# The low-order half of the attention scores as two 64-row matmuls in the two halves of the array

## The chip, the cores and the metric

The kernel runs on one core of a Trainium2 chip. The metric is the time of one execution on the device, in microseconds (us). A run of the kernel before is compared with runs of the changed kernel on the same chip; the profile is a trace of one execution. TensorE is called PE in the rows, its weight loads PEld, VectorE is DVE, ScalarE is ACT, GpSimd is POOL, and SP is the engine that issues most DMAs.

## The reference, cut to what matters

Three stages in a row: an attention with pooled queries, a mixture of eight experts with one expert for each token, and a gated feed-forward layer. The change touches the first alone.

```
B, H, S, D = 4, 8, 1152, 64
q_pool = q.reshape(B, H, S // 2, 2, D).mean(axis=3)        # 576 queries a head
scores = 1.0 / np.sqrt(D) * np.matmul(q_pool, k.transpose(0, 1, 3, 2))   # 576 x 1152
attn   = softmax(scores)                                   # over the 1152 keys
out    = np.matmul(attn, v)
```

## The kernel before

**Pairs and tiles.** The 32 heads are worked in 16 pairs. The 576 queries of each head are four tiles of 128 rows and a rest of 64; the two rests share a ninth tile. So a pair has nine score tiles: 0 to 3 of its first head, 4 to 7 of its second, and tile 8 (`TC`) with 64 rows of each. The 1152 keys are two halves of 512 columns (`h` 0 and 1) and a remainder of 128.

**Parts.** Each fp32 number is split into a high and a low part (fp32r), and a product is made from products of parts. For the scores, `kq_t` holds for each head 19 chunks of 128 columns: nine of keys, five of queries' high parts, five of queries' low parts. Its 128 partitions are two times 64: the keys' high parts lie in partitions 0 to 63 and their low parts in 64 to 127, and the query chunks stand in both halves alike. A score bank of 128 x 512 is then two matmuls over 128 rows in `scores` (L792): queries high by [keys high; keys low], then queries low by the same. Tile 8 has four a bank, two for each head. The remainder goes to bank R in the same way (`scores_rem`, L805). Three banks `S` hold the 18 halves of a pair in turn.

**Other work of a pair.** Transposes of the exponentials `probs` into three banks `T` (L694), from which ACT takes the high part `p_hi` (L514) and DVE the low part `p_lo` (L657); products of both with the values into bank O (L761, for tile 8 L770); groups of transposes of the next-but-one pair's keys and queries (`raw_k`, `q_sum`; also L694), whose parts ACT and DVE put into `kept_rows`; transposing matmuls of the result (L725). For each score half DVE takes a row maximum (L578), for each tile the negated maximum of all three parts (L591), then ACT takes the exponential with the row sum (L538).

**What sets the order.** All is written out by hand. `UNITS` is a list of 27 steps of a pair: b, a and c are transposes of `probs`, g the groups, x the results. `SCORES_AT`, `MAXIMA_AT` and `EXP_AT` say for each tile behind which step PE, DVE and ACT do its scores, maxima and exponentials. Every engine goes through the list in order. The products of a step come three steps behind its transposes. Before a half is written, PE waits until the exponential that read the same bank three halves earlier is done. SP's queue brings the parts from `kept_rows` to `kq_t` by `copy_parts` (L295, L297, L299: six DMAs a pair), then loads the keys, queries and values of the pair after next, then stores results.

The experts' gate logits, behind the attention, are the one place with small arrays: matmuls of 128 rows by 32 columns (L1353), and of 32 rows by 128 columns (L1363), between transposes (L1329).

Of the kernel before, what the change touches and what calls it, by code (L numbers as in the profile page):

```python
# [4 lines left out]
F32 = mybir.dt.float32  # L5
# [7 lines left out]
P = 128  # L13
# [48 lines left out]
def attention(nc, q, k, v, w_gate, w_out_gate, w1, x_dram, xs_dram, ys_dram, shared):  # L62
# [17 lines left out]
    B, H, SK, D = k.shape  # L80
# [4 lines left out]
    CH = SK // P  # L85
    QT = SQ // P
    REM = SQ - QT * P
    TILES = 2 * QT + 1
# [7 lines left out]
    HEAD = (CH + 2 * QC) * P  # L96
# [8 lines left out]
    SR = 3  # L105
# [4 lines left out]

    UNITS = [
# [3 lines left out]
    ]  # L115
    SCORES_AT = [(26, 26), (2, 2), (4, 5), (7, 8), (12, 13), (17, 17), (19, 20), (21, 22), (23, 24)]
    MAXIMA_AT = [(25, 25), (2, 2), (3, 4), (7, 8), (12, 13), (16, 16), (18, 19), (20, 21), (22, 23)]
    EXP_AT = [(0, 2, 2), (4, 4, 4), (7, 8, 8), (11, 11, 13), (16, 16, 17), (18, 19, 20), (21, 21, 21), (22, 23, 23), (25, 25, 25)]

    assert X_LOADS[X_EARLY - 1][1] * P <= (B - 1) * SQ and (B - 1) * HP <= LAST - 1  # L120
    assert w1.shape[2] == PIECE
# [51 lines left out]
    with ctx:  # L173
# [68 lines left out]
        KQ_DMAS, X_DMAS, COPIES = 6, 3, 3  # L242
        assert X_DMAS * PAIRS + 1 == X_STORES and x_out.shape[1] == TILES * D

        def sum_col(tile, part):
# [23 lines left out]
        with nc.Block() as block:  # L269

            @block.sync
            def _(sp):
# [18 lines left out]
                def copy_parts(par):  # L291

                    for h in range(2):
                        src, at = parts[h * D:h * D + D].bitcast(F32), h * HEAD
                        sp.dma_start(kq_t[par][0:D, at:at + HEAD].bitcast(F32), src[:, 0:LO_K]  # L295
                                     ).then_inc(kq_copied[h], 16)
                        sp.dma_start(kq_t[par][D:P, at:at + CH * P].bitcast(F32), src[:, LO_K:LO_K + CH * P]  # L297
                                     ).then_inc(kq_copied[h], 16)
                        sp.dma_start(kq_t[par][D:P, at + CH * P:at + HEAD].bitcast(F32), src[:, CH * P:LO_K]  # L299
                                     ).then_inc(kq_copied[h], 16)  # L300

                def store(p, kind):

# [387 lines left out]
            def _(pe):  # L691
# [82 lines left out]
                def operands(par, tile):  # L774

                    heads = (0, 1) if tile == TC else (tile // QT,)
                    at = CH + (QT if tile == TC else tile % QT)
                    return [(kq_t[par][:, h * HEAD + (at + part * QC) * P:h * HEAD + (at + part * QC + 1) * P], h)
                            for h in heads for part in range(2)]

                def scores(p, par, tile, h, opening=False):

                    if not (opening and 2 * tile + h < SR):

                        pe.wait_ge(exp_done, 2 * TILES * p + 2 * tile + h - SR + 1)
                    if tile in (0, QT) and h == 0:

                        pe.wait_ge(kq_copied[tile // QT], 16 * COPIES * (p + 1))
                    ops = operands(par, tile)
                    for n, (w, head) in enumerate(ops):  # L790
                        at = head * HEAD + h * 512
                        last = nc.tensor.matmul(S[(2 * tile + h) % SR][:, :], w, kq_t[par][:, at:at + 512],  # L792
                                                start=(n == 0), stop=(n == len(ops) - 1))
                    last.then_inc(s_ready, 1)

                def scores_rem(p, par, tile, opening=False):

# [11 lines left out]
                def body(p, par, kind):  # L809
                    j = 0  # L810
                    for n, step in enumerate(UNITS):
                        if step in steps(kind):
                            fill(p, par, kind, j, step)
                            done = lagged(kind, j)
                            if done is not None and is_prob(done):
                                products(p, par, kind, j - LAG, done)
                            j += 1
                        for tile in (*range(1, TILES), 0):
                            if kind == "tail" or (kind == "last" and tile == 0):
                                continue  # L820
                            of = (p, par) if tile else (p + 1, 1 - par)
                            opening = kind == "first" and tile > 0
                            if SCORES_AT[tile][0] == n:
                                scores(*of, tile, 0, opening)
                            if SCORES_AT[tile][1] == n:
                                scores(*of, tile, 1, opening)
# [10 lines left out]
                for g in range(GROUPS):  # L837
# [4 lines left out]
                scores(0, 0, 0, 0, True)  # L842
                scores(0, 0, 0, 1, True)
                scores_rem(0, 0, 0, True)
                over_pairs(pe, body)

# [997 lines left out]
```

## Time and profile before

| | us |
|---|---|
| three runs, lowest, median, highest | 1476.31, 1480.16, 1483.12 |
| the profiled execution | 1476.28 |
| its span, first to last instruction | 1474.5 |
| busy in the span: PE | 1377.8 |
| busy in the span: DVE | 873.2 |
| busy in the span: ACT | 638.4 |

The attention fills the first 600 us or so of the span. A matmul's duration in the rows is longer than the distance to the next, since matmuls are pipelined: how much time one takes on PE is read from start to start. The mean granted clock of TensorE was 0.981 of full speed, and 1.00 in the attention.

### The profile page before, as it was taken

To read this page: it belongs to the slowest core of one execution; us is meant where nothing else is said; L and a number is where in the kernel's file an instruction comes from. 1 tells how busy PE (TensorE), PEld (TensorE's weight loads), DVE (VectorE), ACT (ScalarE), POOL (GpSimd) and SP (SyncE) were. 2 spreads that over 40 slices of the span, in tenths; PEclk is the share of its full clock that TensorE was granted. 3 is DMA by queue.
4 is the path that set the end of the run, shared out by engine and by line. 5 is a ranking of instruction groups with operands and counts; after the bars stand their busy time and mean duration, and the time that the engine had idled before them with its cause. 6 is when DMAs were issued, how large, how long until landed. Compare 5 with 4: busy or idle time off the path is not lost. (4 is left out here: it accounts for less than half of the span.)

```text
span 1474.5 us, 24891 instructions
## 1 busy us (share of the span) xinstructions
PE 1377.8 (93%) x7733; PEld 1195.3 (81%) x7734; DVE 873.2 (59%) x1658; ACT 638.4 (43%) x1549; POOL 345.2 (23%) x241
## 2 busy tenths in 40 slices
PE   3999999999999999739978999998999999999998
PEld 2788888888888888537767787887999999999997
DVE  2899999999999998673443444445632323223232
ACT  2888888788888887532034102004411111111111
POOL 3122222222222220279179205022101010100000
PEclk9999999999999999969998999999999999999999
DMA  7566666666666764356256313114400000000000
GB/s 164 124 139 139 138 138 142 146 144 145 145 149 145 195 132 153 101 193 247 88 199 233 116 43 107 43 57 142 150 32 15 29 15 17 26 0 21 0 22 22
DMA packets 127931, 156.85 MB, mean 106 GB/s; under 512 B 47633, under 2 KB 86545, under 8 KB 125841
## 3 DMA queue, kind: packets, MB, share of 16 engines
q1 hardware_dynamic: 111968, 114.35, 30.8%
q10 hardware_dynamic: 12880, 31.99, 6.5%
q0 software_dynamic: 3040, 9.96, 2.0%
q8 instruction: 25, 0.41, 0.1%
q14 instruction: 18, 0.14, 0.0%
HBM read 87.33 MB, written 29.10 MB: 79 GB/s over the span
## 5 line engine op out<-in xcount | busy, mean ns | idle before, releaser
L514 ACT ACTIVATE p_hi<-ps_t 128x512 fp32r<-128x512 f32 (+1 forms) x336 | 194.3, 586 | 69.1 <-PE ps_t L694 64.7
L657 DVE TENSOR_TENSOR p_lo<-ps_t,p_hi 128x512 fp32r<-128x512 f32 (+1 forms) x336 | 216.9, 666 | 12.4 <-ACT p_hi L514 7.8
L578 DVE TENSOR_REDUCE maxima<-ps_s 128x1 f32<-128x512 f32 x288 | 193.7, 686 | 41.5 <-PE ps_s L792 37.7
L538 ACT ACTIVATE probs<-ps_s,neg_max 128x512 f32<-128x512 f32 x288 | 198.6, 690 | 44.1 <-DVE neg_max L591 43.9
L792 PE MATMUL ps_s<-kq_t 128*128 128x512 f32 x640 | 199.7, 414 | 13.6 <-DMA kq_t<-kept_rows 9.5
L694 PE MATMUL ps_t<-ident,probs 128*128 128x128 f32 x1296 | 198.5, 274 | 1.4 <-DVE kept_rows L569 0.8
L1026 POOL TENSOR_TENSOR w_parts<-raw_w,w_parts 128x1024 fp32r<-128x1024 f32 x64 | 150.9, 2396 | 184.5 <-ACT w_parts L1096 184.4
L694 PEld LDWEIGHTS ps_t<-ident,probs 128*128 128x128 f32 x1296 | 156.0, 140 | 46.3 <-DVE p_lo L657 9.6
L1642 ACT ACTIVATE silu<-ps_g 128x384 f32<-128x384 f32 x72 | 35.4, 491 | 314.6 <-PE ps_g L1748 314.6
L1695 DVE TENSOR_TENSOR silu<-ps_g,silu 128x384 f32<-128x384 f32 x72 | 40.1, 558 | 210.7 <-ACT silu L1642 210.7
L1096 ACT ACTIVATE w_parts<-raw_w 128x1024 fp32r<-128x1024 f32 x64 | 67.1, 1059 | 220.0 <-PE ps_h L1423 104.2
L761 PE MATMUL ps_o<-p_hi,v_hl 128*128 128x512 f32 x288 | 137.7, 478 | 8.4 <-DVE o_sb L598 5.2
L792 PEld LDWEIGHTS ps_s<-kq_t 128*128 128x128 f32 x640 | 114.7, 192 | 37.9 <-DMA kq_t<-kept_rows 9.9
L761 PE MATMUL ps_o<-p_lo,v_hl 128*128 128x512 f32 x288 | 113.6, 394 | 0.0
L1746 PE MATMUL ps_g<-mxt_hi,wg 128*128 128x384 f32 x288 | 97.5, 339 | 2.4 <-DVE mxt_lo L1670 2.4
L1748 PE MATMUL ps_g<-mxt_hi,wg 128*128 128x384 f32 x288 | 97.7, 339 | 0.0
L1747 PE MATMUL ps_g<-mxt_lo,wg 128*128 128x384 f32 x288 | 97.2, 338 | 0.0
L1421 PE MATMUL ps_h<-w_parts,xst_hi 128*128 x200 | 83.0, 415 | 14.6 <-POOL w_parts L1026 11.9
L1748 PE MATMUL ps_v<-mxt_hi,wv 128*128 128x384 f32 x288 | 96.4, 335 | 0.0
L1746 PE MATMUL ps_v<-mxt_hi,wv 128*128 128x384 f32 x288 | 96.4, 335 | 0.0
L1747 PE MATMUL ps_v<-mxt_lo,wv 128*128 128x384 f32 x288 | 96.4, 335 | 0.0
L1446 PE MATMUL ps_y<-w_parts,ht_hi 128*128 x200 | 81.7, 409 | 5.4 <-DVE ht_lo L1289 2.8
(190 smaller groups left out, 2786.5 us busy)
## 6 DMA issues: line engine op xcount, KB each, us to landing
raw_w<-in_moe_w ACTq DMA_DIRECT2D x61, 512.0 KB, 4.1
kq_t<-kept_rows SPq DMA_DIRECT2D x32, 608.0 KB, 6.2
kq_t<-kept_rows SPq DMA_DIRECT2D x32, 320.0 KB, 7.1
raw_k<-in_k SPq DMA_DIRECT2D x32, 288.0 KB, 5.7
raw_v<-in_v SPq DMA_DIRECT2D x16, 576.0 KB, 5.5
kq_t<-kept_rows SPq DMA_DIRECT2D x32, 288.0 KB, 6.5
raw_q<-in_q SPq DMA_DIRECT2D x32, 256.0 KB, 4.1
y_by_slot<-x_out SPq DMA_DIRECT2D x25, 256.0 KB, 2.0
```

The costliest lines, as they stand in the source:

```text
L514: nc.scalar.activation(p_hi[prob_ring(kind, m)][:, 0:w], T[ring(kind, j)][:, 0:w], ACT.Copy).then_inc(hi_ready, 1)
L538: nc.scalar.activation(probs[:, at:at + 512], S[(2 * tile + h) % SR][:, :], ACT.Exp, bias=neg_max[:, tile:tile + 1], accum_out=sums[par][: ...
L578: nc.vector.reduce_max(maxima[:, 3 * tile + h:3 * tile + h + 1], S[(2 * tile + h) % SR][:, :], AX).then_inc(max_done, 1)
L657: nc.vector.tensor_tensor(p_lo[n][:, 0:w], t[:, 0:w], p_hi[n][:, 0:w].bitcast(F32), ALU.subtract).then_inc(t_free, 1)
L694: last = nc.tensor.transpose(dst[:, n * P:(n + 1) * P], src, ident[:, :])
L761: last = nc.tensor.matmul(O[:, :], v_hl[v_par][:, c * P:(c + 1) * P], part[:, :], start=(i == 0 and n == 0), stop=(i == CH - 1 and n == 1))
L792: last = nc.tensor.matmul(S[(2 * tile + h) % SR][:, :], w, kq_t[par][:, at:at + 512], start=(n == 0), stop=(n == len(ops) - 1))
L1026: nc.gpsimd.tensor_tensor(w_part(n, parity, 1, at, PIECE), raw[j % RAW][:, :], w_part(n, parity, 0, at, PIECE).bitcast(F32), ALU.subtract) ...
L1421: nc.tensor.matmul(HB[h][:, :], xh, dyn(0, base, 0, at), start=(c == 0), stop=False)
L1746: nc.tensor.matmul(dst, wh, xh, start=(c == 0), stop=False)
L1747: nc.tensor.matmul(dst, wh, xl, start=False, stop=False)
L1748: last = nc.tensor.matmul(dst, wl, xh, start=False, stop=(c == DC - 1))
```

## The change

The second product (queries' low parts) needs the keys' high parts alone, 64 rows. `kq_t` is laid out anew: for keys 0 to 511 the high parts stay in partitions 0 to 63, for keys 512 to 1151 they lie in 64 to 127, and the low parts opposite. The second product of half 0 is then a matmul over rows 0 to 63 and that of half 1 over rows 64 to 127, into two different banks, issued one behind the other. Both halves of a tile are issued together, and PE's wait for a free bank stands before both. The copies become twelve DMAs a pair. `UNITS` and the three tables have new values. The product of the two low parts, which the kernel before also added, is left out in the 512-column halves.

```diff
     UNITS = [
         ("b", 0), ... ("b", 8),
-        ("g", 0), ("g", 1), ("c", 0), ("c", 1), ("c", 2), ("g", 2), ("a", 0), ("g", 3), ("a", 1),
-        ("a", 2), ("x", 0), ("a", 3), ("x", 1), ("a", 4), ("a", 5), ("a", 6), ("a", 7), ("a", 8),
+        ("g", 0), ("c", 0), ("c", 1), ("g", 1), ("g", 2), ("c", 2), ("g", 3), ("a", 0), ("a", 1),
+        ("a", 2), ("a", 3), ("x", 0), ("a", 4), ("x", 1), ("a", 5), ("a", 6), ("a", 7), ("a", 8),
     ]
-    SCORES_AT = [(26, 26), (2, 2), (4, 5), (7, 8), (12, 13), (17, 17), (19, 20), (21, 22), (23, 24)]
+    SCORES_AT = [26, 2, 5, 8, 12, 15, 17, 20, 23]
...
-                        sp.dma_start(kq_t[par][0:D, at:at + HEAD].bitcast(F32), src[:, 0:LO_K]
-                                     ).then_inc(kq_copied[h], 16)
-                        sp.dma_start(kq_t[par][D:P, at:at + CH * P].bitcast(F32), src[:, LO_K:LO_K + CH * P]
-                                     ).then_inc(kq_copied[h], 16)
-                        sp.dma_start(kq_t[par][D:P, at + CH * P:at + HEAD].bitcast(F32), src[:, CH * P:LO_K]
-                                     ).then_inc(kq_copied[h], 16)
+                        for rows, other, cols in ((slice(0, D), slice(D, P), slice(0, 512)),
+                                                  (slice(D, P), slice(0, D), slice(512, CH * P))):
+
+                            sp.dma_start(kq_t[par][rows, at + cols.start:at + cols.stop].bitcast(F32), src[:, cols]
+                                         ).then_inc(kq_copied[h], 16)
+                            sp.dma_start(kq_t[par][other, at + cols.start:at + cols.stop].bitcast(F32),
+                                         src[:, LO_K + cols.start:LO_K + cols.stop]).then_inc(kq_copied[h], 16)
+                        for rows in (slice(0, D), slice(D, P)):
+                            sp.dma_start(kq_t[par][rows, at + CH * P:at + HEAD].bitcast(F32), src[:, CH * P:LO_K]
+                                         ).then_inc(kq_copied[h], 16)
...
-                def scores(p, par, tile, h, opening=False):
+                def scores(p, par, tile, opening=False):
 
-                    if not (opening and 2 * tile + h < SR):
+                    if not (opening and 2 * tile + 1 < SR):
 
-                        pe.wait_ge(exp_done, 2 * TILES * p + 2 * tile + h - SR + 1)
+                        pe.wait_ge(exp_done, 2 * TILES * p + 2 * tile + 1 - SR + 1)
...
                     ops = operands(par, tile)
-                    for n, (w, head) in enumerate(ops):
-                        at = head * HEAD + h * 512
-                        last = nc.tensor.matmul(S[(2 * tile + h) % SR][:, :], w, kq_t[par][:, at:at + 512],
-                                                start=(n == 0), stop=(n == len(ops) - 1))
-                    last.then_inc(s_ready, 1)
+                    first, second = ops[:len(ops) // 2], ops[len(ops) // 2:]
+                    banks = [S[(2 * tile + h) % SR] for h in range(2)]
+                    for h in range(2):
+                        for n, (w, head) in enumerate(first):
+                            at = head * HEAD + h * 512
+                            nc.tensor.matmul(banks[h][:, :], w, kq_t[par][:, at:at + 512], start=(n == 0), stop=False)
+
+                    for n, (w, head) in enumerate(second):
+                        for h in range(2):
+                            rows, at = slice(h * D, h * D + D), head * HEAD + h * 512
+                            last = nc.tensor.matmul(banks[h][:, :], w[rows, :], kq_t[par][rows, at:at + 512],
+                                                    start=False, stop=(n == len(second) - 1))
+                            if n == len(second) - 1:
+                                last.then_inc(s_ready, 1)
```

In the rows of order, names carry their buffer number, and REGISTER_ALU, L715 and the like only work out the value of a wait. The first place is PE around score tile 3 of a pair in the loop. Before, the two banks are filled behind two different steps:

```order
L694 MATMUL ps_t0<-ident,probs 128x128 x4
L761 MATMUL ps_o<-p_hi6,v_hl0 128x512
L761 MATMUL ps_o<-p_lo6,v_hl0 128x512
L785 REGISTER_ALU
L792 MATMUL ps_s0<-kq_t1 128x512 x2
L706 REGISTER_ALU
L694 MATMUL ps_t1<-ident,probs 128x128 x4
L761 MATMUL ps_o<-p_hi0,v_hl0 128x512
L761 MATMUL ps_o<-p_lo0,v_hl0 128x512
L785 REGISTER_ALU
L792 MATMUL ps_s1<-kq_t1 128x512 x2
```

And with the change, behind one step (L799 is the first product over 128 rows, L804 the second over 64):

```order
L698 MATMUL ps_t1<-ident,probs 128x128 x4
L765 MATMUL ps_o<-p_hi0,v_hl0 128x512
L765 MATMUL ps_o<-p_lo0,v_hl0 128x512
L789 REGISTER_ALU
L799 MATMUL ps_s0<-kq_t1 128x512
L799 MATMUL ps_s1<-kq_t1 128x512
L804 MATMUL ps_s0<-kq_t1 128x512
L804 MATMUL ps_s1<-kq_t1 128x512
```

The four matmuls stay four; they stand together now, and the 64-row ones are enclosed by 128-row work on both sides. The second place is PE from score tile 5 to score tile 6. Before:

```order
L694 MATMUL ps_t1<-ident,probs 128x128 x4
L792 MATMUL ps_s1<-kq_t1 128x512 x2
L785 REGISTER_ALU
L792 MATMUL ps_s2<-kq_t1 128x512 x2
L706 REGISTER_ALU
L694 MATMUL ps_t2<-ident,probs 128x128 x4
L761 MATMUL ps_o<-p_hi0,v_hl1 128x512
L761 MATMUL ps_o<-p_lo0,v_hl1 128x512
L706 REGISTER_ALU
L725 MATMUL ps_t0<-stack2,o_sb 128x64 x4
L785 REGISTER_ALU
L792 MATMUL ps_s0<-kq_t1 128x512 x2
```

With the change, from the last matmul of tile 5 to the first of tile 6:

```order
L804 MATMUL ps_s2<-kq_t1 128x512
L710 REGISTER_ALU
L715 REGISTER_ALU
L698 MATMUL ps_t0<-ident,probs 128x128 x4
L710 REGISTER_ALU
L698 MATMUL ps_t1<-ident,probs 128x128 x4
L774 MATMUL ps_o<-v_hl0,p_hi6 128x256
L774 MATMUL ps_o<-v_hl0,p_lo6 128x256
...
L789 REGISTER_ALU
L799 MATMUL ps_s0<-kq_t1 128x512
```

Between the two tiles there are now two steps (the rows left out are two more pairs of L774), and tile 6 starts with a wait for tile 5's first exponential where before it was for tile 4's second. The third place is SP's queue in one pair, before:

```order
L295 DMA kq_t<-kept_rows 64x2432
L297 DMA kq_t<-kept_rows 64x1152
L299 DMA kq_t<-kept_rows 64x1280
L295 DMA kq_t<-kept_rows 64x2432
L297 DMA kq_t<-kept_rows 64x1152
L299 DMA kq_t<-kept_rows 64x1280
L275 ISA
L275 DMA raw_k<-in_k 128x9x64
```

And with the change:

```order
L298 DMA kq_t<-kept_rows 64x512
L300 DMA kq_t<-kept_rows 64x512
L298 DMA kq_t<-kept_rows 64x640
L300 DMA kq_t<-kept_rows 64x640
L303 DMA kq_t<-kept_rows 64x1280 x2
L298 DMA kq_t<-kept_rows 64x512
...
L303 DMA kq_t<-kept_rows 64x1280 x2
L275 ISA
L275 DMA raw_k<-in_k 128x9x64
```

The bytes are the same; the loads of keys and queries now stand behind twelve DMAs in place of six.

## Rows read from the trace of the kernel before

**Rows 1.** Busy time of each engine in a stretch of the attention
```profile
core 0: us, PE busy (x) PEld busy (x) DVE busy (x) ACT busy (x) POOL busy (x), PEclk, DMA share, GB/s
170.00:240.00 70.00, 69.22 (x447) 58.90 (x445) 64.75 (x134) 57.46 (x158) 13.86 (x12) 1.00 0.63 142
```

**Rows 2.** Timeline of PE, one step with score tile 3: start, us, operation
```profile
208.65 0.60 PE L694 MATMUL ps_t<-ident,probs 128*128 128x128 f32 x4
209.00 0.48 PE L761 MATMUL ps_o<-p_hi,v_hl 128*128 128x512 f32 x1
209.32 0.40 PE L761 MATMUL ps_o<-p_lo,v_hl 128*128 128x512 f32 x1
209.56 0.63 PE L792 MATMUL ps_s<-kq_t 128*128 128x512 f32 x2
210.02 0.60 PE L694 MATMUL ps_t<-ident,probs 128*128 128x128 f32 x4
```

**Rows 3.** Timeline of PE, the same place in two pairs that follow each other
```profile
204.44 0.50 PE L761 MATMUL ps_o<-p_hi,v_hl 128*128 128x512 f32 x1 [0.26 <-DVE o_sb L598]
...
239.92 0.50 PE L761 MATMUL ps_o<-p_hi,v_hl 128*128 128x512 f32 x1 [0.27 <-DVE o_sb L598]
```

**Rows 4.** Timeline of the weight loads, two that follow each other
```profile
208.98 0.19 PEld L761 LDWEIGHTS ps_o<-p_hi,v_hl 128*128 128x128 f32 x1
209.09 0.19 PEld L761 LDWEIGHTS ps_o<-p_lo,v_hl 128*128 128x128 f32 x1
```

**Rows 5.** Timelines of PE, weight loads and DVE, from 32-column to 32-row matmuls
```profile
632.92 0.28 PE L1353 MATMUL ps_h<-w_parts 128*32 128x256 f32 x1
...
633.13 0.18 PEld L1363 LDWEIGHTS ps_l<-stack,h_sb 32*128 32x128 f32 x1 [0.21 <-issue]
...
631.95 0.67 DVE L1168 COPY h_sb<-ps_h 32x512 f32<-32x512 f32 x1
```

**Rows 6.** Timeline of the weight loads, from 32-row matmuls back to full transposes
```profile
628.26 0.30 PEld L1363 LDWEIGHTS ps_l<-stack,h_sb 32*128 32x128 f32 x2
628.59 0.20 PEld L1329 LDWEIGHTS ps_tx<-ident,x_half 128*128 128x128 f32 x2
```

**Rows 7.** Timelines of PE and weight loads, from 32-column matmuls to full transposes
```profile
625.93 0.86 PE L1353 MATMUL ps_h<-w_parts 128*32 128x512 f32 x3
626.63 0.27 PE L1329 MATMUL ps_tx<-ident,x_half 128*128 128x128 f32 x1
...
626.39 0.38 PEld L1329 LDWEIGHTS ps_tx<-ident,x_half 128*128 128x128 f32 x2
```

**Rows 8.** Groups of DVE and ACT in the attention: busy us, mean ns of one
```profile
L578 DVE TENSOR_REDUCE maxima<-ps_s 128x1 f32<-128x512 f32 x288 | 193.7, 686 | 41.5 <-PE ps_s L792 37.7
L591 DVE TENSOR_REDUCE neg_max<-maxima 128x1 f32<-128x3 f32 x144 | 22.5, 156 | 5.0
L538 ACT ACTIVATE probs<-ps_s,neg_max 128x512 f32<-128x512 f32 x288 | 198.6, 690 | 44.1 <-DVE neg_max L591 43.9
```

**Rows 9.** Waits in the attention: engine, line, waited for, us in total, times, longest
```profile
PEld ps_s L792 <- ACT probs L538: 8.4, 8, 1.5
PE ps_s L792 <- ACT probs L538: 3.9, 5, 0.8
```

**Rows 10.** Timeline of PE in the opening of the first pair
```profile
28.89 2.24 PE L792 MATMUL ps_s<-kq_t 128*128 128x512 f32 x4 [0.82 <-ACT probs L538]
31.89 2.24 PE L792 MATMUL ps_s<-kq_t 128*128 128x512 f32 x4 [0.77 <-ACT probs L538]
```

**Rows 11.** Timelines of SP's queue, POOL and PE: copies, their use, the next loads' use
```profile
220.78 0.49 SPq L295 DMA_DIRECT2D kq_t<-kept_rows  x1
...
221.96 2.42 SPq L299 DMA_DIRECT2D kq_t<-kept_rows  x1
...
227.58 2.48 SPq L299 DMA_DIRECT2D kq_t<-kept_rows  x1
...
241.20 0.72 POOL L420 TENSOR_TENSOR q_sum<-raw_q 64x64 f32<-64x64 f32 x2
...
238.13 1.09 PE L792 MATMUL ps_s<-kq_t 128*128 128x512 f32 x4
...
246.88 0.60 PE L694 MATMUL ps_t<-ident,raw_k 128*128 128x128 f32 x4
```

More of the change, by code:

```diff
@@ L112, in attention @@
         ("b", 0), ("b", 1), ("b", 2), ("b", 3), ("b", 4), ("b", 5), ("b", 6), ("b", 7), ("b", 8),
[2 rows of a table removed]
-    ]
-    SCORES_AT = [(26, 26), (2, 2), (4, 5), (7, 8), (12, 13), (17, 17), (19, 20), (21, 22), (23, 24)]
-    MAXIMA_AT = [(25, 25), (2, 2), (3, 4), (7, 8), (12, 13), (16, 16), (18, 19), (20, 21), (22, 23)]
-    EXP_AT = [(0, 2, 2), (4, 4, 4), (7, 8, 8), (11, 11, 13), (16, 16, 17), (18, 19, 20), (21, 21, 21), (22, 23, 23), (25, 25, 25)]
[2 rows of a table added]
+    ]
+    SCORES_AT = [26, 2, 5, 8, 12, 15, 17, 20, 23]
+    MAXIMA_AT = [(25, 25), (2, 2), (5, 5), (8, 8), (11, 11), (15, 15), (17, 17), (19, 19), (23, 23)]
+    EXP_AT = [(0, 2, 2), (4, 5, 5), (7, 8, 8), (10, 11, 11), (13, 15, 15), (17, 17, 17), (19, 19, 20), (21, 22, 23), (24, 25, 25)]
     assert X_LOADS[X_EARLY - 1][1] * P <= (B - 1) * SQ and (B - 1) * HP <= LAST - 1
@@ L241, in attention @@
         x_rows = x_dram.rearrange("(b i) (g c) -> b i g c", b=B, g=HP)
-        KQ_DMAS, X_DMAS, COPIES = 6, 3, 3
+        KQ_DMAS, X_DMAS, COPIES = 6, 3, 6
         assert X_DMAS * PAIRS + 1 == X_STORES and x_out.shape[1] == TILES * D
@@ L778, in operands @@
                     return [(kq_t[par][:, h * HEAD + (at + part * QC) * P:h * HEAD + (at + part * QC + 1) * P], h)
-                            for h in heads for part in range(2)]
-                def scores(p, par, tile, h, opening=False):
-                    if not (opening and 2 * tile + h < SR):
-                        pe.wait_ge(exp_done, 2 * TILES * p + 2 * tile + h - SR + 1)
-                    if tile in (0, QT) and h == 0:
+                            for part in range(2) for h in heads]
+                def scores(p, par, tile, opening=False):
+                    if not (opening and 2 * tile + 1 < SR):
+                        pe.wait_ge(exp_done, 2 * TILES * p + 2 * tile + 1 - SR + 1)
+                    if tile in (0, QT):
                         pe.wait_ge(kq_copied[tile // QT], 16 * COPIES * (p + 1))
                     ops = operands(par, tile)
-                    for n, (w, head) in enumerate(ops):
-                        at = head * HEAD + h * 512
-                        last = nc.tensor.matmul(S[(2 * tile + h) % SR][:, :], w, kq_t[par][:, at:at + 512],
-                                                start=(n == 0), stop=(n == len(ops) - 1))
-                    last.then_inc(s_ready, 1)
+                    first, second = ops[:len(ops) // 2], ops[len(ops) // 2:]
[11 more added lines that the diff above has]
+                                last.then_inc(s_ready, 1)
                 def scores_rem(p, par, tile, opening=False):
@@ L822, in body @@
                             opening = kind == "first" and tile > 0
[L823 to L826, printed above, removed]
+                            if SCORES_AT[tile] == n:
+                                scores(*of, tile, opening)
                                 if tile % QT == 0:
@@ L841, in _ @@
                     group(g, T[g % TR]).then_inc(t_filled, 1)
-                scores(0, 0, 0, 0, True)
-                scores(0, 0, 0, 1, True)
+                scores(0, 0, 0, True)
                 scores_rem(0, 0, 0, True)
```

## The prediction, written before the changed kernel ran

> **What bounds the kernel now.** I read the busy times by stretch first. In the attention PE is busy 69.22 of 70 us, DVE 64.75 and ACT 57.46, at the full clock [rows 1]. So PE sets the pace and DVE is only 7% behind it: whatever PE gives up, at most that share can be gained. Then the timeline of PE at one place of two pairs, for the period: 239.92 - 204.44 = 35.48 us a pair [rows 3], 16 pairs. Then a single step, for what an operation occupies. The two score matmuls start at 209.56 and the next work at 210.02, so a 512-column matmul costs 0.23 us; a step of four transposes and two products runs from 208.65 to 209.56, 0.91 us [rows 2]. A full weight load follows another after 0.11 us [rows 4], and it lies under the matmul that streams meanwhile. That is why 0.23 is the whole price of a matmul: its weights are there when its turn comes. Last I read what PE waits for: the exponentials hold a score matmul up by 8.4 us on the weight loads and 3.9 us on the matmuls in the whole attention [rows 9]. This is little, so a change of the order alone has almost nothing to give.
>
> **What the change removes.** Of the 40 score matmuls of 512 columns a pair, 20 are second products. If the two of a couple stream at the same time, a tile of 0 to 7 needs three slots in place of four (0.23 us less) and tile 8 two couples in place of four matmuls (0.46 less): 2.3 us a pair, 37 us in all. This is the most that it can bring.
>
> **What it adds on PE: the switch.** The 64-row matmuls stand between 128-row work, nine times a pair. The attention of before has no such switch, but the gate logits have. There the last 32-column matmul starts at 632.92; the next load, of 32 rows, needs `h_sb`, which is done at 631.95 + 0.67 = 632.62, so nothing is waited for, and yet it starts at 633.13 [rows 5]. Elsewhere the next load starts together with the matmul. So it came 0.21 late, and its 0.11 of loading lies open behind that. Streaming starts at 633.24, where the 0.11 spacing of these 256-column matmuls would have given 633.03: entering costs about 0.20 us. On the way back the last 32-row loads start at 628.26 and 0.11 later, the first full one should follow at 628.48 and comes at 628.59 [rows 6]: 0.11 late, and here too the load then lies open, where behind a 512-column matmul it would be hidden. So leaving costs 0.11 + 0.11 - 0.02 = 0.20 us. The lower reading: the second full load follows the first after only 0.20 - 0.14 = 0.06, so the open load may be 0.06, and leaving 0.15. The control is the change from 32 columns to the full array, both over 128 rows: the load starts at 626.39, which is when the third matmul of the row starts, and nothing is late [rows 7]. What costs is a change in the number of rows, not any change of shape.
>
> **Inside a couple.** The second 64-row matmul needs its own load. No row shows two row halves at work. From above: no overlap at all, 0.46 for the couple. From below: both start together, 0.23. I take the load of the second behind that of the first, 0.11 [rows 4], so 0.34, since nothing streams under it after the switch and loads of 32 rows follow each other in the same 0.11 as full ones [rows 6]. The Trainium skill (TensorE: Matmul & The Clock Gate, Part 3) has matmuls of different row groups start about 4 ns apart, with the load of one under the matmul of the other; no row here shows it. By it the couple is 0.23 and the sum below would be 16 us smaller.
>
> **Sum for PE.** Tile 0 to 7 before: 4 x 0.23 = 0.92. After: 0.46 + 0.20 + 0.34 + 0.20 = 1.20, so +0.28; with the lower leaving price 1.15. I take +0.25. Tile 8 before: 1.84. After: 0.92 + 0.20 + (0.46 + 0.11) + 0.20 = 1.89, +0.05. A pair: 8 x 0.25 + 0.05 = 2.05 us, 16 pairs: +33 us. Lowest (couple 0.23, leaving 0.15): 8 x 0.12 - 0.11 = 0.85 a pair, +14 us. Highest (no overlap): 9 x 0.40 = 3.6, +58 us. Nothing hides it, since PE is the bound.
>
> **What it adds in waits.** PE now waits before tile t for the first exponential of tile t-1, where it waited for the second of t-2. Behind that wait stands all of PE's queue: the transposes that feed ACT and DVE. Counted from the start of the last 64-row matmul, the banks are ready after about 0.39 (the duration of such a matmul), then two maxima and the negated maximum, 2 x 0.69 + 0.16 = 1.53, then the exponential, 0.69 [rows 8], and three hand-overs of about 0.1: 2.9 us. PE's own work until the next tile's scores is 0.23 + 0.20 and three steps of 0.91: 3.2 us. This fits, barely, for tiles 1 to 3. From tile 5 to tile 6 there are only two steps, a0 with no product and a1 with the six of c2: eight transposes at 0.09 and six 256-column products at 0.12, about 1.5 us with the 0.43 some 2.0: PE waits 0.9 us. I take 0.8 us a pair in 15 pairs, 12 us; bounds 0 (if DVE and ACT are ahead) and 20 (if the other tiles miss too). In the opening the chain runs bare: two tiles' halves there follow each other after 31.89 - 28.89 = 3.0 us [rows 10]; with both halves at once it is 0.46 + 0.20 + 0.11 + 2.9 = 3.7, three or four times: +2 us.
>
> **Copies.** The same bytes in twelve DMAs. They are issued from 220.78 and the last ends being issued at 230.06, and are wanted at 238.13; the loads behind them give `q_sum` at 241.92, wanted at 246.88 [rows 11]. Issuing costs 0.5 us where the queue is free; six more are 3 us, and the slack is 5 us. Cost nothing; without that cover it would be what is beyond 5 us.
>
> **Total.** 33 + 12 + 2 = 47 us on the profiled execution of 1476.28 (a span of 1474.5 and 1.8 around it). The median of the runs, 1480.16, stands 4 above it. So I predict 1525 us, 3% slower.
>
> **Rivals.**
> (1) *The switch costs nothing in the attention*, and the change is faster. It decides from the point at which entering and leaving together cost less than the 0.12 (load behind load) to 0.23 us that the couple saves. Then a tile gives 0.12 to 0.23 and tile 8 0.35 to 0.46: 21 to 37 us over the 16 pairs, less 0 to 14 of waits, about -22: 1458 us. For it: the switch was seen at a few places with small matmuls, not with 64 rows of fp32r. Against it: both directions show it, and nothing else was waited for there. The Trainium skill (TensorEngine Tiling (Array Packing), Key Properties) says that changing the tiling mode drains the engine; rows 5 and 6 agree, and this takes a tenth from this rival's chance. DVE, at 93%, would let through nearly all of it. Chance 0.17.
> (2) *Switch and saving cancel*, as with leaving at 0.05 and a couple of 0.23: 1474 to 1486. Chance 0.06.
> (3) *The two halves do not overlap*: +58 and the waits, about +72, 1552 us. For it: no row shows an overlap. Chance 0.10, on the side of slower.
> (4) *The twelve DMAs make the loads late.* Some issues take 2.4 us [rows 11]; were all six new ones so, SP would be 14 us later and the first group 9 us late in each pair, +140 us. Against it: those long issues came with the bytes in flight, and the bytes are the same. Chance 0.02.
> The forecast: 0.65, with a range of its own from 1494 (14 + 0) to 1560 (58 + 20 + 2).
>
> **Numbers.** A measurement of this kernel tells about 0.5% from no change, 7 us. Faster 0.17, same 0.06, slower 0.77. The range reaches down to 1461, into rival 1 but without its better half, and up to 1556, short of the extreme of rival 3: some 0.2 is left out.
>
> **What would show it.** Right: in the trace after, behind each couple of 64-row matmuls the next full load starts about 0.3 us after the second's start and not with it; the load of the first 64-row matmul starts some 0.3 us behind the last full one's start; a tile's scores take 1.15 to 1.20 us from start to the next work's start; the pair's period is about 38.2 us; the second matmul of a couple starts 0.11 behind the first; PE waits for ACT before tile 6, about 0.8 us; DVE's busy share falls to some 86%. Wrong: if the four matmuls of a tile take 0.8 us or less, the switch is free and rival 1 holds; if couples are 0.46 apart, rival 3; if PE waits for `q_sum` or `kq_t`, rival 4; if the waits for the exponentials exceed 1.3 us a pair, the term of the waits is too small.

## The result and the profile after

The changed kernel is slower: 1520.29 us (median of 4 runs, 1516.14 to 1522.04) against 1479.99 before, a ratio of 1.0269 (1.0238 to 1.0301). The forecast was 1525. The profiled execution took 1516.14 us, 39.9 more than that of before.

Busy times of the engines in the stretch of [rows 1]:

```profile
core 0: us, PE busy (x) PEld busy (x) DVE busy (x) ACT busy (x) POOL busy (x), PEclk, DMA share, GB/s
170.00:240.00 70.00, 67.89 (x418) 49.92 (x417) 61.79 (x127) 54.45 (x149) 11.46 (x11) 1.00 0.54 129
```

All engines are less busy, PE too. It did not only get more to do; it also waits. The period, from the scores of tile 6 in two pairs that follow each other (timeline of PE):

```profile
201.00 0.73 PE L799 MATMUL ps_s<-kq_t 128*128 128x512 f32 x2 [0.77 <-ACT probs L542]
...
238.57 0.73 PE L799 MATMUL ps_s<-kq_t 128*128 128x512 f32 x2 [0.77 <-ACT probs L542]
```

238.57 - 201.00 = 37.57 us a pair, where [rows 3] gave 35.48: 2.09 more. Both rows carry a wait for ACT of 0.77 us; on the weight loads it is 0.97. This is the place with only two steps between tiles 5 and 6. Fifteen periods hold 31 of the 40 us; the rest came in the opening, below. Tile 6 is not the only place. The weight loads of tiles 2 and 3 of the next pair wait too:

```profile
222.21 0.30 PEld L799 LDWEIGHTS ps_s<-kq_t 128*128 128x128 f32 x2 [0.50 <-ACT probs L542]
226.30 0.30 PEld L799 LDWEIGHTS ps_s<-kq_t 128*128 128x128 f32 x2 [0.50 <-ACT probs L542]
```

With 0.17 at tile 7 and 0.15 at tile 0 (212.92) these are 2.3 us of waits for the exponentials in each pair. The kernel before has none there (170 to 310 us).

One tile, on PE and then on its weight loads:

```profile
204.84 0.63 PE L799 MATMUL ps_s<-kq_t 128*128 128x512 f32 x2
205.40 0.50 PE L804 MATMUL ps_s<-kq_t 64*128 64x512 f32 x2
205.83 0.65 PE L698 MATMUL ps_t<-ident,probs 128*128 128x128 f32 x4
206.24 0.48 PE L765 MATMUL ps_o<-p_hi,v_hl 128*128 128x512 f32 x1
```

```profile
204.73 0.30 PEld L799 LDWEIGHTS ps_s<-kq_t 128*128 128x128 f32 x2 [0.17 <-ACT probs L542]
205.40 0.19 PEld L804 LDWEIGHTS ps_s<-kq_t 64*128 64x128 f32 x2 [0.36 <-issue]
205.83 0.42 PEld L698 LDWEIGHTS ps_t<-ident,probs 128*128 128x128 f32 x4 [0.25 <-issue]
```

Three things are to be seen here. First, the two 64-row loads take 0.19 us together, as long as one, and the two 64-row matmuls 0.50, where the median of a single one is 0.497: the two start 3 ns apart and occupy one slot of 0.23. Second, the 64-row loads start at 205.40, which is 0.33 after the start of the second 128-row matmul (204.84 + 0.23), and the load engine waited for nothing that the profile shows ("issue"). Third, the next full load starts at 205.83, which is 0.99 us after the first score matmul. From that load to the product behind the four transposes it is 0.41, where [rows 2] had 0.35, so 0.06 more belongs to the switch. A tile costs 0.99 + 0.06 = 1.05; before it was two halves of 210.02 - 209.56 = 0.46, together 0.92. Tile 8 has four full matmuls and two couples, then the remainder:

```profile
208.50 1.18 PE L799 MATMUL ps_s<-kq_t 128*128 128x512 f32 x4
209.61 0.73 PE L804 MATMUL ps_s<-kq_t 64*128 64x512 f32 x4
210.28 0.66 PE L818 MATMUL ps_r<-kq_t 128*128 128x128 f32 x4
210.78 0.41 PE L698 MATMUL ps_t<-ident,probs 128*128 128x128 f32 x2
```

The same place in the changed kernel with all second products over 128 rows (a run below):

```profile
204.50 1.17 PE L799 MATMUL ps_s<-kq_t 128*128 128x512 f32 x4
205.51 1.08 PE L804 MATMUL ps_s<-kq_t 128*128 128x512 f32 x4
206.43 0.56 PE L818 MATMUL ps_r<-kq_t 128*128 128x128 f32 x4
206.82 0.62 PE L698 MATMUL ps_t<-ident,probs 128*128 128x128 f32 x4
```

To the transposes behind it, tile 8 takes 210.78 - 208.50 = 2.28 us with couples and 206.82 - 204.50 = 2.32 with full matmuls. Two couples pay for one switch in and out, with about 0.05 left over; one does not pay for it.

What the engines waited for in the attention:

```profile
PEld ps_s L804 <- issue: 52.9, 142, 0.7
PEld ps_s L799 <- ACT probs L542: 49.7, 78, 2.9
PE ps_s L799 <- ACT probs L542: 24.3, 25, 2.4
PEld ps_r L818 <- issue: 12.8, 44, 0.4
```

The first is the way into 64 rows, about 0.37 us each time. The second answers to [rows 9]: 8.4 us at 8 places are now 49.7 us at 78, of which 16 us lie in the first 90 us. The opening, which answers to [rows 10]:

```profile
29.83 1.22 PE L799 MATMUL ps_s<-kq_t 128*128 128x512 f32 x2 [1.78 <-ACT probs L542]
34.15 1.22 PE L799 MATMUL ps_s<-kq_t 128*128 128x512 f32 x2 [2.38 <-ACT probs L542]
```

A tile now follows the other after 4.3 us in place of 3.0. The first matmuls on the result (L725 before, L729 after) come at 80.67 before and at 90.69 after: 10 us are lost by then. All this runs at TensorE's lower clock: the profile gives the granted clock after the change as 0.50 from 20 to 40 us, the lower of its two levels (1.2 GHz), and two score matmuls take 1.22 us there and 0.73 later. Those of before take 1.22 too until the tile at 34.90, although the profile lists 1.00 for that stretch, so the 1.00 stated for the attention of before does not hold in its opening. The first score matmuls at the higher clock start at about 39 us before and at 42.8 after; from 20 to 40 us PE was busy for 12.9 us before and for 9.3 after.

### The profile page after: what moved, and what is told of

Read it like the earlier page. It is cut to its first block and busy times, and to the rows that moved or that the text cites. A ratio compares the mean times of both kernels' runs of the same rounds, so it can differ in the third digit from the quotient of the medians.

```text
span 1514.3 us, 24889 instructions
## 1 busy us (share of the span) xinstructions
PE 1400.3 (92%) x7733; PEld 1150.9 (76%) x7734; DVE 874.6 (58%) x1658; ACT 640.0 (42%) x1549; POOL 345.4 (23%) x241
## 5 line engine op out<-in xcount | busy, mean ns | idle before, releaser
L582 DVE TENSOR_REDUCE maxima<-ps_s 128x1 f32<-128x512 f32 x288 | 185.1, 685 | 44.4 <-PE ps_s L804 42.2
L698 PE MATMUL ps_t<-ident,probs 128*128 128x128 f32 x1296 | 195.0, 277 | 0.4 <-DVE p_lo L661 0.4
L698 PEld LDWEIGHTS ps_t<-ident,probs 128*128 128x128 f32 x1296 | 148.7, 140 | 45.3 <-issue 19.1
L799 PE MATMUL ps_s<-kq_t 128*128 128x512 f32 x320 | 109.4, 431 | 35.5 <-ACT probs L542 24.3
L408 POOL TENSOR_TENSOR v_hl<-raw_v,zeros 128x1152 fp32r<-128x1152 f32 x16 | 42.3, 2643 | 251.5 <-PE ps_o L774 251.3
L799 PEld LDWEIGHTS ps_s<-kq_t 128*128 128x128 f32 x320 | 51.5, 191 | 63.3 <-ACT probs L542 49.7
```

The source lines that it names most:

```text
L582: nc.vector.reduce_max(maxima[:, 3 * tile + h:3 * tile + h + 1], S[(2 * tile + h) % SR][:, :], AX).then_inc(max_done, 1)
L698: last = nc.tensor.transpose(dst[:, n * P:(n + 1) * P], src, ident[:, :])
L799: nc.tensor.matmul(banks[h][:, :], w, kq_t[par][:, at:at + 512], start=(n == 0), stop=False)
```

## The experiments

**Theory.** The loss has two parts: the switch between 128 and 64 rows costs PE more than the couple gives back, and one wait for two banks, with a new order around it, makes the score chain late. **Rivals.** The switch is the whole loss; the order or the twelve copies are; or the common start of a couple is nominal. The first three runs go from the kernel before to the changed one in steps. Gains and losses in us are taken from the ratios, since the kernel before ran anew beside each group of runs.

**The order alone.** The kernel before with the new step list and tables:

```diff
-    SCORES_AT = [(26, 26), (2, 2), (4, 5), (7, 8), (12, 13), (17, 17), (19, 20), (21, 22), (23, 24)]
+    SCORES_AT = [(26, 26), (2, 2), (5, 5), (8, 8), (12, 12), (15, 15), (17, 17), (20, 20), (23, 23)]
```

> The kernel before with the new step list and tables alone: each half still has its two 128-row products and its own wait, one half right behind the other. Theory (the loss is the row switch, 0.13 us a tile net, plus the wait for both banks at once): the order itself costs little, 1480 to 1488 us. Rival (the new order is what costs, since maxima and exponentials sit badly in it): 1500 us or more, with the waits for ACT before tile 6 near 1 us a pair, as in the changed kernel.

Measured: 1488.8 us, ratio 1.0055 (1.0032 to 1.0079), a loss of about 8 us and just above the range given. Between theory and rival, near the theory: the order costs something. In its waits the second half, now right behind the first, meets its bank in use. At tile 6 this is 0.73 us in each pair (188.71 and 224.84 on the weight loads), so most of the 0.97 seen there in the changed kernel comes with the order:

```profile
PEld ps_s L792 <- ACT probs L538: 22.4, 27, 1.5
```

**Order and joint wait.** The changed kernel with 128 rows in the second product, and the copies of before:

```diff
-                            last = nc.tensor.matmul(banks[h][:, :], w[rows, :], kq_t[par][rows, at:at + 512],
+                            last = nc.tensor.matmul(banks[h][:, :], w, kq_t[par][:, at:at + 512],
```

> The changed kernel with the second product over all 128 rows and the copies of before: no row switch, no couples, but both halves of a tile issued together behind one wait. Theory: it loses the 0.13 us a tile that switch and couple cost net, 8 x 0.13 - 0.08 = 0.96 us a pair, so about 1505 us; the waits for the exponentials stay. Rival (the switch is the whole loss): 1480 us. Second rival (the switch is repaid in full by the couples and the joint wait is the whole loss): 1520 us.

Measured: 1510.2 us, ratio 1.0208 (1.0181 to 1.0235). Without a single 64-row matmul three quarters of the loss are there. This refutes the rival that the switch is all. It is also 5 us above the size that the theory gave: of what switch and couple cost net on PE's timeline, a part does not reach the time. The waits are nearly those of the changed kernel:

```profile
PEld ps_s L795 <- ACT probs L538: 50.2, 69, 2.7
```

**The new layout with 128 rows.** The same edit on the changed kernel with its own layout and twelve copies.

> The changed kernel with the second product over all 128 rows, but with the new layout and its twelve copies. Theory: the copies are hidden, so it equals the run with the copies of before within 3 us, about 1505 us. Rival (the twelve DMAs make loads late): over 5 us slower than that run.

Measured: 1509.26 us, ratio 1.0203 (1.0173 to 1.0234), 0.9 us from the run before it: the copies are hidden. In the changed kernel `q_sum` is ready at 219.72 and the groups that use keys and queries start at 227.40, so by the reading of [rows 11] there is more slack than the 5 us of before, not less:

```profile
219.01 0.71 POOL L424 TENSOR_TENSOR q_sum<-raw_q 64x64 f32<-64x64 f32 x2
...
227.40 0.66 PE L698 MATMUL ps_t<-ident,raw_k 128*128 128x128 f32 x4
```

**Both of a couple in the same half.** The changed kernel with the layout of before:

```diff
-                            rows, at = slice(h * D, h * D + D), head * HEAD + h * 512
+                            rows, at = slice(0, D), head * HEAD + h * 512
```

> The changed kernel with the copies of before and both 64-row matmuls of a couple in partitions 0 to 63: the switches stay, the two can't stream at once. Theory (in the changed kernel the two start 3 ns apart and share one slot of 0.23 us): each of ten couples a pair becomes 0.23 longer, 2.3 us a pair, so 1520 + 34 = about 1553 us, a little less where a wait hides part. Rival (the common start in the records is nominal and the halves stream one behind the other already): 1520 us.

Measured: 1551.1 us, ratio 1.049 (1.0458 to 1.0523), 31 above the changed kernel; 34 were expected. The timeline of PE and of the loads at one tile:

```profile
206.44 0.73 PE L800 MATMUL ps_s<-kq_t 64*128 64x512 f32 x2
207.10 1.11 PE L814 MATMUL ps_r<-kq_t 128*128 128x128 f32 x8
```

```profile
206.44 0.29 PEld L800 LDWEIGHTS ps_s<-kq_t 64*128 64x128 f32 x2 [0.37 <-issue]
```

The two matmuls take 0.73 and their loads 0.29, where they took 0.50 and 0.19 in two halves. So the overlap is real and full, and worth 0.23 us a couple on PE's timeline. The wait for "issue" ahead is the same 0.37: it belongs to the number of rows, not to the halves. That the total came so near the 34 us is in part chance, as the table behind the runs shows: only 24 us lie in the pairs.

**The couples in the old order.** The changed kernel with the step list, maxima and exponentials of before, and `SCORES_AT = [26, 2, 5, 8, 13, 17, 20, 22, 24]`.

> The changed kernel (couples, joint wait, twelve copies) with the step list, maxima and exponentials of before; a tile's scores stand where its second half stood. Theory: the new order was needed for the joint wait; the switch stays, and waits of ACT and DVE grow, 1525 to 1550 us. Rival (the new order is itself a loss): 1510 us or less.

Measured: 1587.21 us, ratio 1.0716 (1.0689 to 1.0742), far beyond what was expected. The old tables ask for a tile's first maximum a step ahead of its second half; DVE, strictly in order, stands there until the couple is done:

```profile
DVE maxima L582 <- PE ps_s L804: 143.1, 90, 10.1
```

So with couples and one wait the old tables, with a tile's scores where its second half stood, do not serve, and the new order saves 67 us against them; the 8 us of the order alone are small beside that.

**Tile 6 a step later.**

```diff
-    SCORES_AT = [26, 2, 5, 8, 12, 15, 17, 20, 23]
+    SCORES_AT = [26, 2, 5, 8, 12, 15, 18, 20, 23]
```

> The changed kernel with the scores and maxima of tile 6 one step later (18 in place of 17), so that three steps lie between tiles 5 and 6. Theory (a wait of 1.04 us a pair stands before tile 6, since only two steps cover the chain of maxima and exponential): the wait shrinks, by up to 15 us in all, but tile 7 then comes two steps behind tile 6, so part of it comes back there: 1508 to 1520 us. Rival (the waits are not of the place but of ACT and DVE being full): 1520 us or more.

Measured: 1533.0 us, ratio 1.0353 (1.0321 to 1.0386), 13 us slower than the changed kernel. A miss. The wait before tile 6 is smaller (0.33 in place of 0.77), but a new one of 0.85 stands before tile 7:

```profile
206.32 0.73 PE L799 MATMUL ps_s<-kq_t 128*128 128x512 f32 x2 [0.33 <-ACT probs L542]
...
210.75 0.73 PE L799 MATMUL ps_s<-kq_t 128*128 128x512 f32 x2 [0.85 <-ACT probs L542]
```

Together 1.18 in place of 0.77: 0.4 us a pair, 6 us in 15 pairs, so these two waits are about half of the 13 us, and 3 us came in the opening. The rest was not traced. The nine tiles are a chain that is nearly as long as the pair; a tile that is delayed hands the delay on.

**No second product.** The changed kernel without the second products of the 512-column halves.

```diff
-                            nc.tensor.matmul(banks[h][:, :], w, kq_t[par][:, at:at + 512], start=(n == 0), stop=False)
-
-                    for n, (w, head) in enumerate(second):
-                        for h in range(2):
...
-                            if n == len(second) - 1:
-                                last.then_inc(s_ready, 1)
+                            last = nc.tensor.matmul(banks[h][:, :], w, kq_t[par][:, at:at + 512], start=(n == 0),
+                                                    stop=(n == len(first) - 1))
+                        last.then_inc(s_ready, 1)
```

> The changed kernel without the second products of the 512-column halves (the queries' low parts are left out of them): no 64-row matmul, no switch, 20 matmuls fewer a pair. Theory: PE does 0.46 us less a tile than with four full matmuls, 4.6 us a pair, but DVE, 32.9 us of work a pair, and the chain of nine tiles hold the period at 33.5 to 35 us, so 1445 to 1475 us: what a couple without any switch cost could at most have brought was not 37 us. Rival (PE alone bounds): a period of 31 us, about 1405 us.

Measured: 1487.68 us, ratio 1.0046 (1.003 to 1.0062). Even the range of the theory was too low. In 140 us of the attention:

```profile
170.00:310.00 140.00, 127.45 (x806) 100.83 (x806) 127.23 (x264) 112.42 (x309) 29.34 (x24) 1.00 0.58 140
```

PE and DVE are both at 91%: neither bounds alone. What is left is the chain through maxima, exponentials and the wait for two banks; that it holds both is argued, not shown. Even with no second product at all, in this order and with this wait the kernel does not beat the one before, so free couples would not have either.

**The switch alone.** In the kernel before, its order and waits as they were:

```diff
+                        rows = slice(0, D) if h == 1 and n == 1 and tile < TC else slice(0, P)
-                        last = nc.tensor.matmul(S[(2 * tile + h) % SR][:, :], w, kq_t[par][:, at:at + 512],
+                        last = nc.tensor.matmul(S[(2 * tile + h) % SR][:, :], w[rows, :], kq_t[par][rows, at:at + 512],
```

> The kernel before, its order and waits untouched; only the second product of half 1 of tiles 0 to 7 is over rows 0 to 63, alone, so that nothing can share its slot: two switches a tile, eight tiles. Theory (entering 0.21 us, leaving 0.15 us, PE bound): 8 x 0.36 = 2.9 us a pair, 16 pairs, 1480 + 46 = 1526 us. Rival (a switch costs no more than 0.1 us, and the changed kernel lost its time elsewhere): under 1495 us.

Measured: 1514.23 us, ratio 1.0192 (1.0145 to 1.0239), 28 us at the ratio where 46 were expected. At one half, PE and its loads:

```profile
219.77 0.82 PE L793 MATMUL ps_s<-kq_t 128*128 128x512 f32 x2
220.52 0.66 PE L694 MATMUL ps_t<-ident,probs 128*128 128x128 f32 x4
220.93 0.48 PE L761 MATMUL ps_o<-p_hi,v_hl 128*128 128x512 f32 x1
```

```profile
219.54 0.19 PEld L793 LDWEIGHTS ps_s<-kq_t 128*128 128x128 f32 x1
220.09 0.18 PEld L793 LDWEIGHTS ps_s<-kq_t 64*128 64x128 f32 x1 [0.36 <-issue]
```

From 219.77 to 220.52 is 0.75, and 0.06 more behind it: 0.81 against 0.46, so 0.35 for one switch in and out, as the theory had it. Eight of them are 2.8 us a pair, but the result matmuls of two pairs start at 198.60 and 235.87, a period of 37.27, only 1.8 longer than before. One of the 2.8 us fell into short waits that PE had before anyway. In the kernel before, a product waited 0.27 for `o_sb` [rows 3]; in this run none does. Other waits hide in the overlap of the records. The first product behind four transposes starts 0.35 us after the first of them when nothing holds it. Over the steps seen whole in 120 to 540 us, these distances are 0.98 us a pair longer than that before, of which only 0.38 is recorded as idle time, and 0.29 us in this run (not counting the 0.06 behind a 64-row matmul). So 0.7 of the missing microsecond is found.

**One wait, the first half finished first.** The run with the order alone, with one wait for both banks.

```diff
-                    if not (opening and 2 * tile + h < SR):
-                        pe.wait_ge(exp_done, 2 * TILES * p + 2 * tile + h - SR + 1)
+                    if h == 0 and not (opening and 2 * tile + 1 < SR):
+                        pe.wait_ge(exp_done, 2 * TILES * p + 2 * tile + 1 - SR + 1)
```

> The new order with full 128-row halves, one finished behind the other (so the first half is ready early), but one wait for both banks ahead of them. The run with the order alone took 1488.8, the one with joint wait and interleaved halves 1510.2. Theory (what costs 21 us is that PE stands before the first half until the bank of the second is free): about 1505 us. Rival (it is the later end of the first half, 0.46 us, that delays maxima and all behind them): about 1490 us.

Measured: 1508.23 us, ratio 1.0179 (1.0143 to 1.0215). Against 1.0055 for the order alone, the joint wait costs 1.2%, some 18 us; that the first half ends later (1.0208 with the halves interleaved) adds at most 0.3%, inside the intervals. The theory holds. Here, as in the changed kernel, the score loads wait long for exponentials: 8.9 us in 170 to 310 us (7.9 in the changed kernel), where the order alone has 3.1.

**Two waits in the changed kernel.** Each bank's wait ahead of its own first product:

```diff
-                    if not (opening and 2 * tile + 1 < SR):
-                        pe.wait_ge(exp_done, 2 * TILES * p + 2 * tile + 1 - SR + 1)
...
                     for h in range(2):
+                        if not (opening and 2 * tile + h < SR):
+                            pe.wait_ge(exp_done, 2 * TILES * p + 2 * tile + h - SR + 1)
                         for n, (w, head) in enumerate(first):
```

> The changed kernel with its couples, but each bank has its own wait ahead of its first product. Theory (joint wait costs): PE starts the first half earlier, 3 to 10 us less than the changed kernel's 1520, about 1513 us. Rival (the couple must wait for both banks anyway, and the chain through maxima and exponential sets the pace): no difference, 1518 to 1522 us.

Measured: 1509.76 us, ratio 1.0183 (1.0149 to 1.0217). By the ratios this is 0.8% or 12 us better than the changed kernel, somewhat more than the 3 to 10 expected, and still behind the one before. It also shows that the steps do not simply add up. With two waits, the order alone stands at 1.0055 and the order with couples at 1.0183: 1.3%, 19 us. With one wait, full rows stand at 1.0203 and couples at 1.0269: 0.7%. In a couple the first half's 64-row product stands behind the wait for the second bank even here; a run with interleaved full rows and two waits, which would tell that share from the switch, was not made.

**Before without second products.**

```diff
                     ops = operands(par, tile)
+                    ops = ops[::2]
```

> The kernel before, its order and waits, without any second product of the 512-column halves (queries' low parts left out there): 20 matmuls of 0.23 us a pair fewer, 4.6 us. With the new order and joint wait the same omission took 1487.7 us at a period of 35.8 us a pair. Theory (there the joint wait and the chain bound, here DVE with 32.9 us of work a pair is the next bound): a period of 33.3 to 34.3 us, 1445 to 1462 us. Rival (the score chain over three banks bounds near 35 us with any order): 1472 us or more.

Measured: 1458.34 us, ratio 0.9839 (0.9807 to 0.9872). Result matmuls of two pairs start at 216.36 and 250.23, a period of 33.87, as the theory had it, and DVE is at 96%:

```profile
170.00:310.00 140.00, 131.57 (x850) 108.07 (x849) 134.10 (x278) 118.00 (x328) 29.47 (x24) 1.00 0.63 146
```

So 74 us of matmul slots (16 x 4.6) are worth 24 us: with DVE at 96% there is little more to gain.

**Openings and pairs of all runs.** Read from the traces, one execution each: when the first score matmuls run at the higher clock (by their durations), when the first and the last result matmul start, and their distance divided by 15. The last pair is shorter than the others, so this is a little below the period.

| run | higher clock from, us | first result | last result | a pair |
|---|---|---|---|---|
| before | 39 | 80.7 | 605.0 | 34.95 |
| order alone | 39 | 82.5 | 616.7 | 35.61 |
| one wait, first half first | 41 | 87.1 | 632.4 | 36.35 |
| order and joint wait | 41 | 87.5 | 634.0 | 36.43 |
| new layout, 128 rows | 42 | 88.4 | 634.8 | 36.43 |
| changed kernel | 43 | 90.7 | 645.2 | 36.97 |
| two waits | 42 | 87.2 | 633.7 | 36.43 |
| switch alone | 50 | 86.7 | 637.6 | 36.73 |
| tile 6 later | 58 | 93.6 | 657.5 | 37.59 |
| same half | 61 | 99.1 | 677.5 | 38.56 |
| no second product | 57 | 87.6 | 615.5 | 35.20 |
| before, no second | 46 | 80.8 | 582.6 | 33.45 |
| couples in the old order | 50 | 92.5 | 714.2 | 41.45 |

The runs that go in steps reach the higher clock within 39 to 43 us and can be compared as they are. The attention's 40 us are then, in order: the order 12, the joint wait 16, interleaving (both halves' first products ahead of both second ones) and copies 2, switch and couple 10. Of the opening's 10 us these are 2, 5, 1 and 2. In other runs the lower clock lasts up to 18 us longer than in the changed kernel, and what they lose by the first result is in part that: of what the same half costs over the changed kernel, 24 us lie between the results (1.6 us a pair, not the 2.3 of the timeline) and 8 in the opening; of the switch alone, 27 and 6 over the kernel before. The run without second products stays behind the kernel before in the pairs too (35.20 against 34.95), so what is said of it does not hang on its opening. What makes the clock rise early or late was not tested.

## Why the prediction was right, by its steps

**The sign and size** were right: 1525 forecast, 1520.29 measured. (The sum of 47 us gives 1523 on the profiled execution and 1527 on the median; 1525 lies between.) The parts were not of the sizes given. By the steps of the experiments, in ratios: order 0.55%, joint wait and interleaving 1.5%, copies nothing, switch and couple 0.7%.

**Entering 0.20, leaving 0.20 or 0.15: right.** The 64-row loads start 0.33 behind the last full matmul's start and, as the prediction took it, need their 0.11 before anything streams; the slot would have been 0.23, so entering costs 0.21. It holds for 512 columns and 64 rows as for the small matmuls of [rows 5]. Of leaving the lower reading was right: 1.05 - 0.46 - 0.21 - 0.23 = 0.15 a tile. The division between the two is worked out so; what is shown by itself, by the switch run, is 0.35 for both.

**The couple at 0.34: wrong.** The term was taken from the load spacing of one half; two halves load and stream together, and it is 0.23. The rule of the Trainium skill (TensorE: Matmul & The Clock Gate, Part 3: different row groups start about 4 ns apart) agrees with this trace: two matmuls of 0.497 start 3 ns apart and take 0.50. The prediction should have given that rule more weight, since the rows it preferred were all of one half. With both corrections a tile costs +0.13, next to the lower end that the prediction had kept (+0.12), and PE's extra work is 8 x 0.13 - 0.05 = 0.99 us a pair, 16 us in all, in place of 33.

**"Nothing hides it, since PE is the bound": too strong.** Of those 16 us only 11 reached the time (1520.3 against 1509.3), and in the switch run 28 of 46. PE at 99% busy still held about a microsecond a pair of small waits.

**The waits at 12 us, and 2 in the opening: too small.** This step failed in "this fits, barely, for tiles 1 to 3". The wait before tile 6 was found where and as long as computed (0.9 forecast, 0.97 on the loads), though 0.73 of it is there with the order alone. But the loads wait 0.50 at tile 2 and at tile 3 as well, 2.3 us a pair in all in place of 0.8, and so beyond the 1.3 that the prediction had named as its sign of being wrong. The chain of 2.9 us supposed that DVE and ACT turn to a tile's scores at once. From tile 5 to 6 they do, and it takes 201.00 - 197.99 = 3.0 us. From tile 1 to 2 it takes 222.21 - 218.37 = 3.8. There each engine, working in order, had something else first:

```profile
218.37 0.19 PEld L804 LDWEIGHTS ps_s<-kq_t 64*128 64x128 f32 x2 [0.36 <-issue]
...
218.87 0.68 DVE L602 COPY o_sb<-ps_o 128x512 f32<-128x512 f32 x1
219.47 1.28 DVE L582 TENSOR_REDUCE maxima<-ps_s 128x1 f32<-128x512 f32 x2
220.78 0.16 DVE L595 TENSOR_REDUCE neg_max<-maxima 128x1 f32<-128x3 f32 x1
...
220.89 0.60 ACT L518 ACTIVATE p_hi<-ps_t 128x512 fp32r<-128x512 f32 x1 [0.72 <-PE ps_t L698]
221.38 0.68 ACT L542 ACTIVATE probs<-ps_s,neg_max 128x512 f32<-128x512 f32 x1
```

DVE copies the result before the maxima (0.6 us late), and ACT takes a `p_hi` before the exponential (0.4 late). A margin of 0.3 us left no room for either. In the opening the loss was 10 us in place of 2. The prediction's 3.7 us from tile to tile took the matmuls at the higher clock's price, and it is 4.3 at the lower one; of the 1.3 over the 3.0 of before, the one wait holds 0.9 (3.86 where the first half is finished first), interleaving 0.2 (4.03), the couple 0.3. The two errors, 22 too much on the switch (33 against 11) and about 15 too little on the waits and the order (14 against 29), offset each other; the good total owes that much to luck.

**The rivals.** That the switch is free (0.17) is refuted by the switch run, and its gain of 21 to 37 us was overrated: the run of before without second products bounds any such gain at 24 us, and the changed order leaves none. No overlap (0.10) is refuted by the run with both in one half. The late loads (0.02) did not come. DVE's share was forecast at 86% and is 88% (61.79 of 70).

**Open.** What makes up the 8 us of the order alone was seen only as more waits for the exponentials (22.4 against 8.4 us), not taken apart. Couples for tile 8 alone were not tried; by its rows they are worth 0.05 us a pair, under 1 us in all, less than a measurement tells. Nor was the clock in the opening taken apart.

## What to carry to other kernels

Matmuls over 64 rows in the two halves of the array do share one slot, but each visit to that mode costs about 0.36 us, so one couple of 512 columns (0.23 saved) loses and two do little more than break even: collect several couples behind one switch (by these numbers; no run here does it), or leave it. Before an optimisation of the busiest engine, count what its neighbour is at: with DVE 7% behind, taking 4.6 us a pair from PE brought 1.6. An edit that issues two things together where they were apart turns two loose waits into one tight one; here that cost more than the edit itself, and a wait of its own for each bank, placed at its first use, gave 0.8% back. When a chain through other engines is set against a margin, count also what those engines do ahead of it in their own order.

## What the runs showed of the hardware

- Changing the number of rows to fewer (128 to 64, and 128 to 32 together with the columns) holds back the next weight load: it starts 0.33 us after the start of a 512-column matmul and 0.21 after that of a 256-column one ([rows 5]), each about 0.1 beyond that matmul's slot. Changing the number of columns alone (32 to 128, [rows 7]) holds nothing back. The Trainium skill (TensorEngine Tiling (Array Packing), Key Properties) says that a change of tiling mode drains the engine; for rows the trace agrees, at 0.36 us for in and out, and for columns it does not show it.
- Two 64-row loads in different halves take 0.19 us together and 0.29 in the same half; two matmuls 0.50 and 0.73.
- PE can be counted busy for 99% of a stretch and still have a microsecond in 35 to give, since the recorded matmuls overlap: 2.8 us a pair added by the switch alone lengthened the period by 1.8.
- At the start of the attention two 512-column score matmuls take 1.22 us, and 0.73 from some 39 to 61 us on, depending on the run; where the profile's clock column shows the stretch (20 to 40 us of the changed kernel), it is 0.50.
